# Attention, routing and two expert layers on one core: the attention loop on TensorE starts at another place of its cycle, and one product of the search moves

## The reference, cut to what matters

```
for c in range(nc):                                    # 24 chunks of 32 rows
    k_full = concatenate([mem_k, k[l_start:r_end]])    # at most 8 + 56 columns
    a = exp(scores - max); a = a / (sum(a) + 1e-09)
    out[:, :, c_start:c_end] = matmul(a, v_full)
...
logits = x @ w_gate
for idx in argsort(-logits.flatten()):                 # token takes its expert if there is room
    if assigned[tok] >= 0 or counts[e] >= cap: continue
    assigned[tok] = e; counts[e] += 1
for e in range(E):
    out[mask] = relu(x[mask] @ w1[e]) @ w2[e]          # 384 tokens each
...
h = x @ w_in; solu = h * softmax(h)
out = layer_norm(solu) * g_ln @ w_out
```

## Time and profile before

| | us |
|---|---|
| median of three runs | 759.92 |
| the profiled execution, its own time | 760.91 |
| its span | 759.1 |
| attention loop, first scores to last values | about 7 to 110 |
| first search and choice of the first expert | about 114 to 154 |
| eight experts and the end | about 154 to 759 |
| PE busy over the span | 705.1 (93%) |
| PEld / DVE / ACT / POOL busy | 626.4 / 528.4 / 328.0 / 321.4 |
| mean granted clock of PE | 0.948 of full speed |

### The profile page before, as it was taken

One profiled execution on the slowest core, in us unless ns is written; L12 is line 12 of the kernel. 1 busy time (PEld: TensorE's weight loads), 2 busy tenths in 40 slices (PEclk: granted clock), 3 DMA queues, 4 the chain that ended last, 5 costly groups with the idle time before them and its releaser, 6 DMA issues.

```text
span 759.1 us, 17892 instructions
## 1 busy us (share of the span) xinstructions
PE 705.1 (93%) x7122; PEld 626.4 (83%) x7122; DVE 528.4 (70%) x1918; ACT 328.0 (43%) x537; POOL 321.4 (42%) x242
## 2 busy tenths in 40 slices
PE   7899993299999999999999999999999999999992
PEld 5788883289888989898989898889888988899882
DVE  4366757788888788868886888688778877542240
ACT  1255556242465146414741474157315722571360
POOL 2011105684375156515751574167317731762011
PEclk8599995599999999999999999999999999999997
DMA  8689997350331032103321331132113301330001
GB/s 341 209 307 371 386 339 277 97 167 2 98 112 55 29 123 100 65 26 120 104 77 33 106 113 56 55 98 98 56 57 112 111 30 56 111 111 29 1 15 41
DMA packets 24925, 89.09 MB, mean 117 GB/s; under 512 B 3360, under 2 KB 3360, under 8 KB 24864
## 3 DMA queue, kind: packets, MB, share of 16 engines
q0 software_dynamic: 13056, 46.14, 18.7%
q1 hardware_dynamic: 11808, 42.17, 15.0%
HBM read 75.71 MB, written 12.58 MB: 116 GB/s over the span
## 4 chain that ended last, share of the span: by engine, by line
PE 86%; DVE 9%; issue 2%; ACT 1%; POOL 0%; DVEq 0%; POOLq 0%
PE banks L563 24%; PE banks L565 22%; PE banks L564 22%; PE banks L486 3%; PE banks L443 3%; PE banks L467 3%; PE banks L592 2%; PE bank L453 2%; PE bank L478 2%; DVE inv L1228 2%; PE banks L576 1%; DVE ul L1252 1%; DVE flips L1060 1%; PE bank L556 1%; PE bank L505 1%
## 5 line engine op out<-in xcount | busy, mean ns | idle before, releaser
L1413 POOL TENSOR_TENSOR wl<-raw,wh 128x1024 fp32r<-128x1024 f32 x60 | 146.6, 2444 | 30.6 <-ACT wh L780 29.4
L1407 POOL DMA_INDIRECT raw<-w,w_idx x60 | 67.3, 1121 | 151.8 <-DVE w_idx L1123 110.8
L563 PE MATMUL banks<-xh,wh 128*128 128x384 f32 x256 | 90.2, 352 | 2.2 <-DVE xl L1259 2.2
L563 PE MATMUL banks<-hh,wh 128*128 128x384 f32 x256 | 90.2, 353 | 0.0
L565 PE MATMUL banks<-xh,wl 128*128 128x384 f32 x256 | 86.3, 337 | 0.0
L565 PE MATMUL banks<-hh,wl 128*128 128x384 f32 x256 | 86.3, 337 | 0.0
L564 PE MATMUL banks<-xl,wh 128*128 128x384 f32 x256 | 85.9, 336 | 0.0
L564 PE MATMUL banks<-hl,wh 128*128 128x384 f32 x256 | 85.9, 335 | 0.0
L563 PE MATMUL banks<-wout_h,uh 128*128 128x512 f32 x192 | 79.1, 412 | 0.0
L563 PE MATMUL banks<-win_h,yh 128*128 128x512 f32 x192 | 77.4, 403 | 0.0
L565 PE MATMUL banks<-wout_h,ul 128*128 128x512 f32 x192 | 75.4, 393 | 0.0
(11 more groups left out here) (202 smaller groups left out, 1573.7 us busy)
## 6 DMA issues: line engine op xcount, KB each, us to landing
unit<-qk_in SPq DMA_DIRECT2D x24, 768.0 KB, 6.3
vr<-v_in SPq DMA_DIRECT2D x24, 520.0 KB, 5.1
x_rows<-x_keep SPq DMA_DIRECT2D x20, 256.0 KB, 5.2
prep_first<-w_in SPq DMA_DIRECT2D x4, 512.0 KB, 7.1
x_rows<-x_sb SPq DMA_DIRECT2D x4, 256.0 KB, 4.5
prep_first<-w_out SPq DMA_DIRECT2D x2, 512.0 KB, 9.0
prep_rest<-w_out SPq DMA_DIRECT2D x2, 512.0 KB, 10.2
raw<-w,w_idx POOLq DMA_INDIRECT x60, 4.3
```

The costliest lines, as they stand in the source:

```text
L563: nc.tensor.matmul(bank, stat_h, mov_h, start=first, stop=False)
L1407: gp.indirect_dma_start(stage(s, c), None, table, bass.IndirectOffsetOnAxis(ap=w_idx[:, c % WCH:c % WCH + 1], axis=0))\
L1413: gp.tensor_tensor(wl[:, c % WCH, :], stage(s, c), wh[:, c % WCH, :].bitcast(F32), ALU.subtract)\
```

## The change

`step` is written in another order. Before: scores, probabilities, gate, x_T, values. Now: x_T and values of the tile one earlier, then scores, probabilities, gate. The cyclic order of the five pieces is the same; the loop's start and end lie elsewhere in it. There is one blank x_T and one blank values more, so BLANK_X and BLANK_XT are one higher, two more memsets stand on DVE, and the numbers in the waits on `pv_ps` and `xT_ps` are one higher. In SP's stream v(2) waits for the first (blank) values, which it did not before. In the three tables the products of the y stage's first group m = 0 stand one place later: behind k = 1 and 6 instead of 0 and 5, in ROUNDS_SECOND 1 and 5 instead of 0 and 4, in ROUNDS_FIRST 5 instead of 4.

```diff
-ROUNDS = rounds_of([[0, 5]], [[2], [2], [3], [], [3], [3], [], [1]], [[2], [4]], [[0, 5], [2, 7], [4], [1, 6]])
+ROUNDS = rounds_of([[0, 5]], [[2], [2], [3], [], [3], [3], [], [1]], [[2], [4]], [[1, 6], [2, 7], [4], [1, 6]])
...
-                if u >= DEEP - 1:
-                    sp.wait_ge(pv_ps, u - DEEP + 2)
+                if u >= DEEP - 2:
+                    sp.wait_ge(pv_ps, u - DEEP + 3)
...
+                if not known or i <= NT + 2:
+                    x_T(i - 1, (r - 3) % DEEP)
+                if not known or i <= NT + 1:
+                    values(i - 1, (r - 2) % DEEP, n)
                 if not known or i < NT:
                     scores(i, r, n)
                 if not known or i <= NT:
                     probs_T(i, (r - 1) % DEEP)
                 gate(i, (r - 3) % DEEP)
-                if not known or i <= NT + 1:
-                    x_T(i, (r - 2) % DEEP)
-                if not known or i <= NT:
-                    values(i, (r - 1) % DEEP, n)
...
+            nc.vector.memset(x_sb[:, 1, :, :, :], 0.0).then_inc(x_ready, 1)
+            nc.vector.memset(pT[:, :, :, :], 0.0).then_inc(pT_sb, BLANK_PT)
+            nc.vector.memset(vr[:, RING - 2 * CPT:RING - CPT, :, :], 0.0).then_inc(v_loaded[DEEP - 2], 16)
+            nc.vector.memset(xT[:, 0, :, :], 0.0).then_inc(xT_sb, BLANK_XT - 1)
             nc.vector.memset(x_sb[:, 2, :, :, :], 0.0).then_inc(x_ready, 1)
-            nc.vector.memset(pT[:, :, :, :], 0.0).then_inc(pT_sb, BLANK_PT)
             nc.vector.memset(vr[:, RING - CPT:RING, :, :], 0.0).then_inc(v_loaded[DEEP - 1], 16)
-            nc.vector.memset(xT[:, 0, :, :], 0.0).then_inc(xT_sb, BLANK_XT - 1)
```

More of the change, by code:

```diff
@@ L51 @@
 KEPT = NT - DEEP
-BLANK_PT, BLANK_X, BLANK_XT, BLANK_SHIFTED, BLANK_GATE = 2, 2, 3, 2, 4
+BLANK_PT, BLANK_X, BLANK_XT, BLANK_SHIFTED, BLANK_GATE = 2, 3, 4, 2, 4
 TG = 12
@@ L90, in rounds_of @@
     return out
-ROUNDS = rounds_of([[0, 5]], [[2], [2], [3], [], [3], [3], [], [1]], [[2], [4]], [[0, 5], [2, 7], [4], [1, 6]])
-ROUNDS_FIRST = rounds_of([[0, 0]], [[2], [2], [2], [3], [3], [3], [3], [3]], [[], []], [[4], [1, 5], [1, 5], [1, 6]])
-ROUNDS_SECOND = rounds_of([[0]], [[], [2], [3], [], [3], [3], [], [1]], [[2], [0, 5]], [[0, 4], [1, 5], [1, 5], [1, 6]])
+ROUNDS = rounds_of([[0, 5]], [[2], [2], [3], [], [3], [3], [], [1]], [[2], [4]], [[1, 6], [2, 7], [4], [1, 6]])
+ROUNDS_FIRST = rounds_of([[0, 0]], [[2], [2], [2], [3], [3], [3], [3], [3]], [[], []], [[5], [1, 5], [1, 5], [1, 6]])
+ROUNDS_SECOND = rounds_of([[0]], [[], [2], [3], [], [3], [3], [], [1]], [[2], [0, 5]], [[1, 5], [1, 5], [1, 5], [1, 6]])
 ROUNDS_NONE = [[[]], [[]] * KF, [[]] * 2, [[]] * KD]
@@ L423, in _ @@
                 store(u)
-            sp.wait_ge(pv_ps, NT + 1)
+            sp.wait_ge(pv_ps, NT + 2)
             for n in range(8):
@@ L751, in _ @@
                     act.wait_ge(pT_ps, i + 1)
-                    if i >= 2:
-                        act.wait_ge(pv_ps, i - 1)
+                    act.wait_ge(pv_ps, i)
                     nc.scalar.activation(pT[:, (i - 1) % 2, :, :].rearrange("p a q -> p (a q)"), PT_PS[:, :], ACT.Copy)\
@@ L760, in _ @@
                 if 2 <= i <= NT + 1:
-                    act.wait_ge(xT_ps, i + 1)
+                    act.wait_ge(xT_ps, i + 2)
                     act.wait_ge(gate_ps, i)
@@ L963, in normalise @@
                 pv = PW[:, :, 0:HP * (D + 1)].rearrange("p a (h d) -> p a h d", h=HP)
-                ve.wait_ge(pv_ps, u + 2)
+                ve.wait_ge(pv_ps, u + 3)
                 nc.vector.tensor_scalar(rs[:, r % 2, :, :], pv[:, :, :, D], 1e-9, None, ALU.add).then_inc(row_sum, 1)
@@ L970, in normalise @@
                     ve.wait_ge(x_kept, u - DEEP + 1)
-                if u >= 2:
-                    ve.wait_ge(xT_ps, u - 1)
+                if u >= 1:
+                    ve.wait_ge(xT_ps, u)
                 nc.vector.tensor_tensor(x_sb[:, u % DEEP, :, :, :].rearrange("p h a d -> p a h d"), pv[:, :, :, 0:D],
```

## The result

The kernel after the change took 747.07 us (median of 4 runs, 746.38 to 747.80). Four runs of the kernel before on the same chip took 759.76 (757.53 to 759.92). The ratio is 0.9841 with a 95% interval of 0.9817 to 0.9866: faster, by 12.7 us. The forecast was 748.0. The profiled execution took 746.67 us, its span 745.0.

The account below looks back on a forecast made before the run. PE, with 86% of the chain, was taken to bound the kernel. Terms -8.5 (start), -1.8 (branch), -3.0 (count products) and +1 (late next) sum to -12.3; forecast 748.0 us, 744 to 752 with the two courses, range 743.5 to 757.5.

Parts of the forecast that it names:

- The start: First pass through the attention loop: shorter instruction stops and earlier clock return, blank work included, -8.5 us.
- two courses: First pass: PE keeps clock 1.00, -10.5 us, or the clock falls at about 14 us and returns at 21 to 28, -6.8.
- The course in which the clock never falls: First pass: PE keeps clock 1.00, seventh scores start at 33.0 us, -10.5 us.
- The start does not improve: First pass: code blocks come as late as before, clock returns at about 41 us; -3.8 us in all, 756.1; chance 0.20.
- the clock stays low until about 41 us: First pass: stops go but groups take 5.6 us at the low clock; -7.2 us in all, 752.7; chance 0.08.
- Slower: First pass: PE gets the 2.4 GHz level back later than before, low to 57 us or beyond; 764 us; chance 0.12.
- The blank group: In front of the first scores: one more blank x_T and values on PE's path, +1.4 us.
- The branch: Loop branch back: 0.51 us of issue wait hides behind the gate; four at full clock, 4 x 0.45 = -1.8 us.
- the gap stays wherever the branch stands: Loop branch back: the gap is code being brought back, so 1.8 + 0.4 us less is won, 750; chance 0.05.
- The count products: Expert y stages: waits in front of the first count product are hidden or covered, -3.0 us.
- What is late next: Behind the loop: DMA-bound stores and weights and the search follow less well, +1 us, bounds 0 and +2.3.

Follow-up runs that it names:

- 2, tables alone: The kernel before with only the three new tables of count products: 756.66 us, ratio 0.9971.
- 3, loads later: The kernel before with every load of v from v(2) on waiting for one more values group: 759.07 us, ratio 1.0015.
- 7, stream shifted: The kernel before with 30 tiny matmuls (60 pairs) behind the warm ones: 759.35 us, ratio 1.0000.
- 1, loop alone: The changed kernel with the three tables of count products as before: 752.42 us, ratio 0.9924 to the kernel before.
- 5, again: The changed kernel run once more, unedited: 749.21 us, ratio 0.9878 to the kernel before.
- 11, again: The changed kernel run a third time, unedited: 748.27 us, ratio 0.9857 to the kernel before.
- 4, qk(2) later: The changed kernel with the load qk(2) issued behind the first blank values: 750.14 us, ratio 0.9908 to the kernel before.
- 6, branch behind x_T: The changed kernel with groups ordered values, scores, probabilities, gate, x_T, one blank values and no blank x_T more: 749.04 us, ratio 0.9886 to the kernel before.
- 8, paced: The changed kernel with qk and v of tile u issued behind the values of group u - 1: 748.01 us, ratio 0.9852 to the kernel before.
- 9, paced, v(1): The changed kernel with paced qk and v loads, v(1) too behind the first blank values: 746.89 us, ratio 0.9826 to the kernel before.
- 10, again: The kernel with paced loads and v(1) behind the first blank values, run once more: 746.41 us, ratio 0.9851 to the kernel before.

## Why the prediction came out right, term by term

Each profile is one execution, and not always one near the median. To show how much is chance, here is what all thirteen have, in us (the turned loop is the new order of the group, in the change and in numbers 1, 4 to 6 and 8 to 11):

| | first scores | stops of the first pass | low in the start | seventh scores | last logits to first expert product | experts |
|---|---|---|---|---|---|---|
| before | 7.04 | 2.45, 2.59, 0.80 | 27.4 | 43.49 | 40.05 | 604.56 |
| 2, tables alone | 6.46 | 2.37, 4.07, 0.52 | 23.9 | 42.27 | 38.95 | 603.36 |
| 3, loads later | 7.04 | 2.35, 0, 2.44 | 30.7 | 43.80 | 40.62 | 605.03 |
| 7, stream shifted | 8.23 | 2.17, 1.43, 0 | 23.9 | 41.79 | 38.85 | 605.76 |
| 1, loop alone | 7.37 | 2.64, 0, 0.48 | 20.5 | 38.51 | 39.47 | 604.90 |
| the change | 8.47 | 2.33, 0, 0 | 6.8 | 34.44 | 37.99 | 602.00 |
| 5, again | 8.34 | 3.01, 0, 0 | 13.6 | 36.94 | 39.07 | 601.95 |
| 11, again | 7.44 | 2.67, 0, 0 | 20.5 | 38.27 | 39.57 | 602.94 |
| 4, qk(2) later | 8.44 | 0.66, 2.28, 0 | 13.7 | 37.20 | 39.01 | 601.96 |
| 6, branch behind x_T | 8.03 | 2.21, 0.77, 0 | 13.6 | 36.97 | 38.15 | 601.83 |
| 8, paced | 7.26 | 2.50, 0, 0 | 17.1 | 37.40 | 37.92 | 602.07 |
| 9, paced, v(1) | 7.41 | 0.19, 1.99, 0 | 3.4 | 32.03 | 39.01 | 601.90 |
| 10, again | 8.19 | 0, 1.99, 0 | 6.8 | 33.56 | 39.23 | 601.46 |

*The start*, forecast -8.5 with two courses of -10.5 and -6.8. The first profile showed -9.05 (43.49 to 34.44), the three of the change -9.05, -6.55 and -5.22, a mean of -6.9. All are counted from the one profile of before; two others with the old loop have 42.27 and 43.80. The mechanism was right in the stops: the first stop inside its bounds of 1.1 to 2.8 but for once (3.01), the second and third within 0 to 1.2 (at 0), a fall of the clock at about 14 and its return at 21 to 28 twice; the third time it came at 32.7, outside. The course in which the clock never falls occurred in no profile. So the term was 1.6 us too good: I took the middle of the two courses where only one of them happens. The argument for the return at 21 to 28 rested on a wrong reading. Before, the clock was said to come back during values and scores, directly behind a gate; it came back at 41.3, at the end of the transposes of probabilities, with the last gate products before it begun at 35.84. So two of three returns fell into that span by luck.

*Its rivals.* "The start does not improve" and "the clock stays low until about 41 us" did not occur: all nine profiles with the turned loop had the clock back by 32.7, all four with the old loop at 39.5 to 45.3. Execution 11 stands between the forecast and the second of them. "Slower" would have wanted the low level until 57 us.

*The blank group*, forecast +1.4. The first profiles have 8.47 against 7.04, +1.43; but over all the first scores start at 7.26 to 8.47 with the turned loop and at 6.46 and 7.04 with the old one (number 7 has its 60 pairs in front). The mean of the nine is 7.88, against 6.85: +1.0. But the warm matmuls in front took from 4.24 to 5.49 us, whatever the loop, and that moves the first scores too. From their end to the first scores it is 1.1 to 1.4 us in the eight profiles with a blank x_T and values, and the scores overlap that end by 0.07 in the old loop: a mean of +1.3, near the forecast.

*The branch*, forecast 4 x 0.45 = -1.8. From the seventh scores to the last transposes of probabilities behind the loop (107.41 before, 96.52 after) it is 63.92 us before and 62.08 after: -1.84. All eight profiles with the change's order have 62.08. The rival, by which the gap stays wherever the branch stands, falls: behind the gate's eight pairs or the four of x_T it is gone, in the change as in number 6. That its 0.45 us are not code that is brought back is told by the count of transfers, not by the move, which could hide either.

The Trainium skill ("Runtime: NRT & Kernel Launch", Instruction fetch mechanics) says that a taken branch forces a fetch if its target isn't in the window of blocks at hand, and puts TensorE's instruction memory at 2048 instructions. The trace agrees with that size: this loop of 4 x 288 = 1,152 matmuls and weight loads and a few more comes back without a wait, and the instruction queue's two transfers between 30 and 110 us both lie behind 90. The same section calls the window two pages; with its blocks of 256 instructions as pages the loop would be larger than the window, and every pass would fetch. The trace shows no such transfer, and the measurement decides.

*The count products*, forecast -3.0. The experts take 601.5 to 602.9 us in the eight profiles with the turned loop and the new tables (mean 602.0) and 604.6 to 605.8 in the four with the old tables (mean 605.1): -3.0. In the first pair it was -2.6. The second y stage was forecast to keep 0.20 us of its 0.73; 0.33 us of idle time is left there.

*What is late next*, forecast +1 with 0 and +2.3 as bounds. This was the wrong sign. Between the last logits and the first expert product the first pair shows 40.05 to 37.99, -2.05. Most of it is the 3.07 us of DVE beside POOL, and that does not belong to the old loop: numbers 2 and 7 keep it and have 0.90 there. Number 3, also with the old loop, has 3.06:

```profile
134.13 4.66 POOL L1390 TENSOR_TENSOR wout_l<-prep_first,wout_h 128x1024 fp32r<-128x1024 f32 x2
133.45 3.06 DVE L1060 TENSOR_SCALAR flips<-digits 96x4 int32<-96x4 int32 x3
```

In both slow cases the three instructions end with one of POOL's: 135.93 beside 135.91, and here 136.51 beside 136.46 (134.13 and half of 4.66). Seven other profiles have two such instructions that take 1.49 to 2.35 us at POOL's first subtraction. So what this stretch costs depends on where the search meets POOL. Over all, the nine profiles with the turned loop have a mean of 38.8, the four others 39.6: -0.8. The stores and weights did not come later relative to the loop. Here I built a term on a slow instance of a row as if it were the rule.

*What I did not see*: the stop of 0.91 us behind the loop, always with 49 of 64 values done. It is 0.37 and 0.64 us in the two repeats of the change and absent in number 1 and before. (In number 6, with its other order, it is 0.21 us with 54 done.)

By the first pair: -9.05 - 1.84, then +1.36 between the last transposes of probabilities and the last logits (107.41 to 114.44 before, 7.03; 96.52 to 104.91 after, 8.39), -2.05, -2.6: -14.2, the difference of the spans (759.1 to 745.0, -14.1). The +1.36 had no term. It is this stop, which is 0.37 us in number 5, and gate products at the low clock (1.88 us, 1.06 in number 5, which has 7.03 us as before); over all profiles the turned loop has 7.6 and the old one 7.1 us there. The medians differ by 12.7 in that series and by 10.3 and 12.1 in the two others. The sum of -12.3 met them partly by luck: a start that was taken 1.6 us too good and an end taken 1.8 us too bad cancel. From the median of 759.92 this sum gives 747.6 and from the profiled execution 748.6; the forecast of 748.0 lies between them.

**What stays open.** Why the clock returns sooner with the turned loop. The sums show what each microsecond costs, not what ends it. From the last idle time in front of PE to the return it took 5.7 to 19.1 us in the thirteen profiles, and in the same program 6.8, 12.8 and 19.1. In eight profiles it took 5.7 to 7.8. It is not the stops' length alone: those of number 7 sum to 3.60 us, those of numbers 4 and 6 to 2.94 and 2.98, and the low level lasted 23.9 against 13.7 and 13.6 us. One thing that the four old loops share, and no turned one, is a wait of 0.27 or 0.28 us at the first branch at the low level; the clock came back 7.3 to 12.7 us behind it. That this wait holds the clock down fits, but no run here sets it alone, so it is argued, not shown.

## What to carry to other kernels

Try a hardware loop's branch behind a few long instructions of the engine that bounds it, not behind many short ones; here turning the cycle cost two blank pieces, 1.3 us once, and saved 0.46 us in each of the passes that could be compared. Read stops of a first pass that no data and no semaphore explain as places in the instruction stream: count instructions to them, look in the DMA view for a transfer of the instruction queue some 2 us before their end, and see which loads were issued before it. Where a stop costs the clock, its price is the time at the low level behind it, several times its own length and different from one execution to the next, so take a mean over several profiles before you put a term on it, and never a single slow instance of a row.

## What the runs showed of the hardware

- A stop keeps its place in the stream when the work is shifted: 60 pairs in front moved two stops by 60 pairs of work, to within one (number 7).
- A stop of the first pass ends 2.2 to 2.6 us (21 of 23 stops) after a transfer of the instruction queue begins to show in windows of 0.2 us (11.8 against 14.29 in the change).
- With fewer loads in front a block of code comes sooner: the first stop ended at 13.49 to 14.84 with all of them (numbers 1, 5, 11 and the change), at 12.59 and 13.25 with 768 KB less (numbers 4 and 8), and at 11.10 with v(1) later as well (number 9; in number 10 it was gone). The same places cost nothing when passed again.
- The granted clock falls to 0.50 between 1.5 us before the end of a stop (12.0 against 13.49 in number 1) and 2.5 us behind it (16.1 against 13.59 in number 2, 19.0 against 16.65 in number 9). In numbers 4, 9 and 10, with a first stop of 0.66 us or less, it held 1.00 until the second one, of 1.99 to 2.28 us, had begun. With PE busy without a gap behind the stop it came back after 6.8 us in one execution of the change and after 19.1 in another. This alone makes 4 to 5 us of the kernel's time, more than the tables gave.
- Three DVE instructions of 4 elements a partition took 3.07 and 3.06 us where they lay wholly beside POOL's operations on 128x1024, and ended within 0.05 us of an end of one (before and number 3). They took 0.90 where they began 0.73 us before POOL's end.
